# Two chained MLPs behind an attention block: GpSimd squares 240 of a unit's 960 columns instead of 192

## The reference

```python
# attention: 32 inducing points attend to x, then x attends to the result
h = mab(I, x)                     # softmax(scale * I x^T) x
x = mab(x, h)                     # softmax(scale * x h^T) h
# first MLP, d_ff = 2048
h = x @ w_in
P = a[0] + a[1]*h + a[2]*h**2 + a[3]*h**3
Q = 1.0 + |b[0]|*|h| + |b[1]|*h**2
x = (P / (Q + 1e-06)) @ w_out
# second MLP, d_ff = 2048
h = x @ w2_in
out = (h * cos(h)) @ w2_out
```

## Time and profile before

| | |
|---|---|
| median of 3 runs | 2550.24 us |
| profiled execution, own time | 2551.46 us |
| its span | 2549.7 us |
| busy TensorE, VectorE, ScalarE, GpSimd | 2526.5 (99%), 2335.5 (92%), 2448.7 (96%), 2102.2 (82%) us |
| granted TensorE clock, mean | 0.996 |
| first MLP | from about 80 to 1420 us |
| second MLP | from about 1420 us to the end |

### The profile page before, as it was taken

One profiled execution on the slowest core, in us unless ns is written; L12 is line 12 of the kernel. 1 busy time (PEld: TensorE's weight loads), 2 busy tenths in 40 slices (PEclk: granted clock), 3 DMA queues, 4 the chain that ended last, 5 costly groups with the idle time before them and its releaser, 6 DMA issues.

```text
span 2549.7 us, 38970 instructions
## 1 busy us (share of the span) xinstructions
PE 2526.5 (99%) x10790; PEld 1812.1 (71%) x10790; DVE 2335.5 (92%) x2866; ACT 2448.7 (96%) x3155; POOL 2102.2 (82%) x1471
## 2 busy tenths in 40 slices
PE   8999999999999999999999999999999999999999
PEld 6566666666666666666666788888888888888887
DVE  5899999999999999999999888888888888888887
ACT  5899999999999999999999999999999999999998
POOL 0588888888888888888888888888888888888886
PEclk9899999999999999999999999999999999999999
DMA  7200000000020000000000000000000000000000
GB/s 220 70 12 8 12 8 12 8 12 8 12 77 13 8 12 8 12 8 12 8 12 1 21 11 10 12 12 12 12 12 12 12 12 12 12 12 12 12 12 16
DMA packets 27816, 48.94 MB, mean 19 GB/s; under 512 B 3352, under 2 KB 12344, under 8 KB 27512
## 3 DMA queue, kind: packets, MB, share of 16 engines
q1 hardware_dynamic: 27768, 48.33, 6.5%
HBM read 18.04 MB, written 12.78 MB: 12 GB/s over the span
## 4 chain that ended last, share of the span: by engine, by line
PE 93%; DVE 3%; issue 2%; DMA 1%; ACT 0%; SPq 0%; POOL 0%; DVEq 0%; POOLq 0%; ACTq 0%
PE bank L1104 24%; PE bank L1272 22%; PE bank L1097 22%; PE bank L1264 21%; PE bank L1113 1%; PE bank L1255 1%; DVE work L831 1%; PE bank L1025 1%; DVE work L825 1%; PE bank L1121 1%; DMA x_ring<-in_x_dram 1%; DVE work L812 0%; PE bank L1034 0%; PE bank L1054 0%; DVE bank L803 0%
## 5 line engine op out<-in xcount | busy, mean ns | idle before, releaser
L485 POOL TENSOR_TENSOR act_lo<-work,act_hi 128x960 fp32r<-128x960 f32 (+1 forms) x413 | 831.3, 2013 | 196.7 <-ACT act_hi L667 196.6
L1104 PE MATMUL bank<-work,v 128*128 128x480 f32 x1664 | 739.5, 566 | 0.0
L1097 PE MATMUL bank<-part_hi,stack_now 96*128 96x480 f32 x2496 | 678.2, 406 | 7.5 <-DVE work L825 3.0
L426 POOL TENSOR_TENSOR work<-work 128x960 f32<-128x960 f32 x278 | 621.6, 2236 | 40.7 <-POOL work L415 5.6
L989 DVE SCALAR_TENSOR_TENSOR work<-work,bank 128x960 f32<-128x960 int32 x416 | 479.3, 1152 | 140.2 <-ACT work L654 139.0
L1097 PEld LDWEIGHTS bank<-part_hi,stack_now 96*128 96x128 f32 x2496 | 437.4, 189 | 219.1 <-DVE work L825 125.4
L803 DVE SCALAR_TENSOR_TENSOR bank<-bank,over_c,work 128x960 f32<-128x960 f32 x416 | 509.0, 1224 | 27.6 <-PE bank L1097 15.7
L995 DVE TENSOR_TENSOR work<-work,bank 128x960 f32<-128x960 f32 x416 | 477.4, 1148 | 0.0
L566 ACT ACTIVATE work<-work,made 128x960 f32<-128x960 f32 x416 | 456.2, 1097 | 4.7 <-POOL work L426 1.3
L1104 PEld LDWEIGHTS bank<-work,v 128*128 128x128 f32 x1664 | 314.1, 189 | 203.8 <-issue 179.2
L654 ACT ACTIVATE work<-bank 128x960 int32<-128x960 f32 x416 | 404.7, 973 | 37.7 <-PE bank L1264 37.7
(11 more groups left out here) (124 smaller groups left out, 3066.1 us busy)
## 6 DMA issues: line engine op xcount, KB each, us to landing
x_group<-tokens_t SPq DMA_DIRECT2D x52, 240.0 KB, 2.2
out_dram<-work SPq DMA_DIRECT2D x52, 240.0 KB, 2.4
x_ring<-in_x_dram SPq DMA_DIRECT2D x28, 240.0 KB, 4.1
work<-in_x_dram SPq DMA_DIRECT2D x24, 240.0 KB, 3.6
w_raw<-in_moe_w_in_dram SPq DMA_DIRECT2D x2, 1024.0 KB, 9.6
stack_now<-first_hi SPq DMA_DIRECT2D x8, 192.0 KB, 3.9
stack_now<-next_hi SPq DMA_DIRECT2D x16, 96.0 KB, 2.2
stack_now<-first_lo SPq DMA_DIRECT2D x4, 192.0 KB, 4.9
```

The lines of the kernel that those rows point to most:

```text
L426: nc.gpsimd.tensor_tensor(quot[k % 3], square[k % 3], abs_h[k % 3], ALU.add).then_inc(den_ready, 1)
L485: nc.gpsimd.tensor_tensor(act2_lo[:, k % 2, w], angle[k % ANGLES][:, w], act2_hi[:, k % 2, w].bitcast(F32), ALU.subtract).then_inc(act2_pa ...
L1097: mm = pe.matmul(place_out[:, t, :], stack_now[:, i, w], part_hi[0:K3, place, :], start=start, stop=stop, skip_group_check=not start)
L1104: mm = pe.matmul(sums, v[:, 2 * u + t, :], g[:, t * GROUP:(t + 1) * GROUP], start=(2 * u + t == 0), stop=(2 * u + t == CHUNKS - 1))
```

## The change

`OWN`, the number of columns of each half of 480 that ScalarE squares, goes from 384 to 360. ScalarE's square becomes 2 x 360 columns in place of 2 x 384, GpSimd's rest 2 x 120 in place of 2 x 96. Each engine has the same instructions in the same order as before, with the same waits.

```diff
@@ -65,7 +65,7 @@
 TINY_BETA, TINY_SIGMA = 2.0 ** -40, 2.0 ** -46
 SPLIT = GROUP
 
-OWN = 384
+OWN = 360
 
 
 HID, MAG, SLOPE, NUM, QUO, DEN = 5, 4, 3, 2, 1, 3
```

## The result

| | before | after |
|---|---|---|
| median of 15 runs each, us | 2550.88 (2548.56 to 2551.76) | 2556.11 (2553.39 to 2557.36) |
| ratio to before, 95% interval | | 1.0019 [1.0012, 1.0026] |
| profiled execution, own time | 2551.46 | 2555.96 |
| its span | 2549.7 | 2554.2 |

The kernel got 5.2 us slower by the medians (3.1 to 6.6 by the interval), which is 0.19%, and 4.5 us slower between the two profiled executions. All of the 4.5 us lies in the first MLP: the last quotient of it ends at 1420.97 us before and at 1425.46 us after, and the second MLP takes the same time.

The account below looks back on a forecast made before the run. The bound was taken to be a loop between VectorE and TensorE in the first MLP. Unit 4's 2.3 + 2.4 and the blocked split's 2.6 made 7.3 us, giving 2557.5, range 2556 to 2559.7 (over all 2550.4 to 2560.2).

Parts of the forecast that it names:

- The price of the rest: GpSimd's rest (L415), grown from 192 to 240 elements, takes 0.108 us more; ends 0.097 and 0.126.
- The square: ScalarE's square (L582), at 0.80 ns an element, ends 0.039 us earlier.
- (a): Most of the rest's added time is hidden: units to spare between rest and product, GpSimd 11% idle.
- (b): Unit 4 of each group: unit 2's denominator ends 0.216 later, unit 4's square 0.176 later; 4.7 us in sum.
- The slack: At unit 4: none in some 13 groups, 0.176 passes; 0.02 and 0.06 in some 25, 0.096 passes.
- (c): Twelve groups where VectorE splits the second MLP's weights: it waits for unit 2's denominator, 0.216 later each; 2.6 us.
- (d): VectorE's normalising of attention (L781) could overlap unit 0's denominator by 0.04 us; taken as nothing.
- A: Slack at unit 4 takes the delay: 0 to 1 us, 2550.8; chance 0.24.
- B: Only (b) or only (c) passes: 2.6 to 4.7 us, 2553.9; chance 0.11.
- C: ScalarE sets the pace, each of 416 units gains 0.039: 16 us faster, 2534; chance 0.05.
- D: Costlier GpSimd rest, (d) biting, or ScalarE staying late within the group: 10 to 12 us, 2561; chance 0.05.

Follow-up runs that it names:

- experiment 2: Two kernels against before (384): first 360 at units 1 and 2 only, 2557.32 us; second 360 everywhere but units 1 and 2, 2550.00 us.
- experiment 1: Kernel before with only GpSimd's rest lengthened (from 360), ScalarE still squaring 384: 2557.22 us, ratio 1.0030.
- experiment 4: Kernel before with OWN raised from 384 to 408: 2550.91 us, ratio 1.0000.
- experiment 6: Kernel before with 408 at units 1 and 2 of each group and 360 elsewhere: 2548.99 us, ratio 0.9991.
- experiment 7: Kernel before with 432 at units 1 and 2 of each group, 384 elsewhere: 2548.41 us, ratio 0.9991.
- experiment 10: Kernel before with the second weight split moved, two sizings: 432 at units 1 and 2, 384 elsewhere, 2547.06 us; 408 there, 360 elsewhere, 2545.61 us.
- experiment 8: Kernel before (384) with each group's second weight split moved four units earlier in VectorE's order: 2545.71 us, ratio 0.9983.
- experiment 5: Kernel before with only ScalarE's square lengthened to 408, GpSimd still from 384: 2553.51 us, ratio 1.0011.

## Why the prediction was right, and what was mis-sized

The forecast was 2557.5, +7.3; measured is +5.2, and +4.5 between the profiled executions. The mechanism is the one that was named, and one price in it was too high. The cost lies below the forecast's own low end of 6.2, and the change isn't shown to be over 0.2%, which had the largest chance. That the time, 2556.11, still lies in the range of 2556 to 2559.7 owes something to luck: the 15 runs of before have a median 0.64 us above the one that the forecast was added to.

**The price of the rest: the step that failed.** "From 192 to 960 elements ... 2.25 ns an element, so +0.108 us", with 0.097 and 0.126 as ends. Measured is +0.080, below the low end. The four sizes now on hand, 144, 192, 240 and 288 columns, take 427, 505, 585 and 667 ns: 1.67 ns a column. I drew a line from a short operation to one five times as long and with two different inputs, and read the price of a small change from it; the middle and the low end came from that long operation, and the high end from the short one's whole duration, so none could have caught a line that is flatter at the short end. The sum with 0.080: late by 2 x 0.080 - 0.042 = 0.118. Third groups 13 x 0.118 = 1.5 (measured 0.117 each). Others 25 x (0.118 - 0.08) = 1.0 (measured 0.055 each, 1.4). Split groups 12 x 0.16 = 1.9 (0.154 each, 1.8). Together 4.4, where the traces show 4.5. The Trainium skill (Perfetto Trace Analysis, GPSIMD Engine Instruction) would have the start-to-start spacing trusted over the spans: the spacing from rest to denominator went from 0.65 to 0.73, the 0.080 that the durations give too, so here spans and spacing agree, and what misled was the slope, by either.

**The square**: -0.042 measured, -0.039 forecast.

**(a) hidden elsewhere**: shown by experiment 2, where the change at the six other units costs nothing.

**(b) the path over unit 4**: shown. Logarithm at the denominator's end, absolute value at the square's end, 1.24 and 1.29 after the quotient. I had expected VectorE's wait as a row of its own. In after it is too short for one (100 and 22 ns); it shows as the idle time of ScalarE ahead of L566, and on VectorE itself as a row only where the lateness is larger: once in experiment 1, twice in the first kernel of experiment 2 and 25 times, over both buffers, at twice the dose.

**The slack**: right in sum, wrong in its reading. I took the third groups to be without slack and the others to have 0.02 and then 0.06. The table says that both have the same floor, 25.486, and that either pays its lateness less some 0.05: 184 - 132 = 52 ns in the third groups, 106 - 57 = 49 in the others, 321 - 265 = 56 and 239 - 185 = 54 at 336 columns. The traces show where it goes: from the end of the quotient of unit 2 to the product of unit 4 it is 0.638 us in the others of before and 0.578 in both kinds of after. In before, the third groups had their 59 ns of lateness, which just used the slack up and cost 0.015. For the change under study the two readings give nearly the same number; for its reverse they don't, and that is why experiments 4, 6, 7 and 10 were expected to gain 0.7 to 1.0 us that wasn't there to be had.

**(c) the blocked split**: shown twice, by 0.72 to 0.88 us here and by experiment 8. Its price was 0.216 in the forecast, two rests, and 0.154 came, of two times 0.080.

**(d) the normalising of attention**: taken at nothing, and it is. It starts at 805.27 while the denominator of unit 0 ends at 805.28; it takes 0.28, and the product follows it by 0.33 as against 0.32 before.

**Rivals.** A (the slack takes it) falls: it needed under 0.08 of lateness and 0.118 came. B (only one part) falls by the table, in which ordinary and split groups each have their share. C falls for this change; for its reverse ScalarE does hold the loop, but at one place in a group, for 2.6 us in experiment 5 where a bound of every unit would be 16. D needed a rest dearer than any row said; it was cheaper. The rest of the misses of experiments 4, 7 and 10 comes from one omission: I had given ScalarE 25.1 of 25.5 us in a group as comfortable, and had looked at its ends at one unit only.

**What stays open.** Why the short operation's slope is 1.67 ns when the line to the long one has 2.25: the two also differ in that L415 multiplies, and reads one tensor for both inputs, where L426 adds two. No run separates length from these.

## What to carry to other kernels

Where three engines are full and wait for each other in a ring, a change of one engine's work is priced unit by unit: find the one unit of a period at which the engines touch without slack, count how many instances of the changed operation lie ahead of it back to back, and look on the other engine for the same kind of point before taking the reverse for a gain. Price a small change of size from operations of nearby size, and, where the trace has none, keep the ends of the range wider than the slope to a much longer operation. Before shifting work between engines, look for an instruction with unusual spread of its duration (0.28 and 0.72 us for the same form): moving it, and its neighbour with the same spread, to another place in the engine's order gained 4.9 us here, about as much as the change under study lost.

## What the runs showed of the hardware that was not expected

- GpSimd's float32 square: 427, 505, 585 and 667 ns for 144, 192, 240 and 288 columns on 128 partitions, against 2236 for a sum of 960.
- A VectorE operation with two SBUF inputs (L950), blocked by a GpSimd denominator, ended 0.15 us after the end of the denominator's record, though it needs 0.28 alone. If it does all of its 0.28 once it is let in, the block is lifted some 0.13 before the recorded end; that is worked out, not seen. The 0.01 of overlap of (d) is in keeping with it. L945, a cast with one input, was blocked in the same way, 0.78 to 0.97 us against 0.28. The Trainium skill (SBUF — State Buffer) has the exclusion last for the whole instruction; by these records it lasts nearly so.
- In this loop a lateness of some 0.05 us at unit 4 costs nearly nothing, taken up by the 0.06 us between quotient and product, and what goes beyond it is paid in full in every group.
- Where ScalarE's copy of y came last, the first matmul that uses it started 0.13 to 0.15 us after the copy's recorded end, in each of four kernels.
